# The first expert tile of a fused attention and mixture-of-experts kernel: nine token blocks read back, three picked by one-hot products

## The reference

```python
def reference(**kwargs):
    # 2 batches x 8 heads x 768 tokens x 64: attention only between tokens of one hash bucket
    attn_out = _attn_ref(q, k, v, proj)
    x = attn_out.transpose(0, 2, 1, 3).reshape(1536, 512)
    x = _moe_ref(x, w_in, w_out, a, b)        # g(x @ w_in) @ w_out, d_ff 2048, g a quotient of polynomials
    return _moe2_ref(x, w_gate, w1, w2)       # below

def _moe2_ref(x, w_gate, w1, w2):             # 8 experts, d_ff 1024, one expert per token
    logits = x @ w_gate
    expert_idx = np.argmax(logits, axis=1)
    probs = softmax(logits)
    for e in range(E):
        mask = expert_idx == e
        h = np.maximum(x[mask] @ w1[e], 0.0)
        out[mask] = probs[mask, e][:, None] * (h @ w2[e])
```

## Time and profile before

| | us |
|---|---|
| median of 3 executions | 814.49 (814.44 to 814.61) |
| the profiled execution | 812.37 |
| its span, first to last instruction | 810.5 |
| PE busy | 776.7 (96%) |
| DVE, ACT, POOL busy | 562.9, 492.6, 456.2 |
| mean granted clock of TensorE | 0.987 |

### The profile page before, as it was taken

One profiled execution on the slowest core, in us unless ns is written; L12 is line 12 of the kernel. 1 busy time (PEld: TensorE's weight loads), 2 busy tenths in 40 slices (PEclk: granted clock), 3 DMA queues, 4 the chain that ended last, 5 costly groups with the idle time before them and its releaser, 6 DMA issues.

```text
span 810.5 us, 13370 instructions
## 1 busy us (share of the span) xinstructions
PE 776.7 (96%) x4279; PEld 688.0 (85%) x4279; DVE 562.9 (69%) x966; ACT 492.6 (61%) x975; POOL 456.2 (56%) x404
## 2 busy tenths in 40 slices
PE   6899999999998999999999999995999999999997
PEld 4799899899996889999999999894788888888886
DVE  4788888888896787887778887975354444544451
ACT  4678878878898898778778877954123224222100
POOL 3335265265157687557647654516895659954810
PEclk9999999999999999999999999995999999999999
DMA  8997987975840850960692040074752727561100
GB/s 193 191 218 168 209 168 168 210 167 130 200 154 21 288 186 0 314 220 1 211 356 86 1 186 23 0 223 169 242 192 74 247 68 248 179 234 28 64 36 19
DMA packets 71842, 123.42 MB, mean 152 GB/s; under 512 B 33342, under 2 KB 36126, under 8 KB 67680
## 3 DMA queue, kind: packets, MB, share of 16 engines
q1 hardware_dynamic: 64176, 90.71, 41.9%
q10 hardware_dynamic: 5056, 25.56, 9.4%
q0 software_dynamic: 2544, 6.31, 2.1%
HBM read 60.26 MB, written 34.24 MB: 117 GB/s over the span
## 4 chain that ended last, share of the span: by engine, by line
PE 88%; ACT 5%; issue 3%; DVE 3%; POOL 1%; DMA 1%; POOLq 0%; SPq 0%; ACTq 0%; DVEq 0%
PE ps L1405 7%; PE ps L1493 5%; PE ps L1495 5%; PE ps L1494 5%; PE ps L1527 5%; PE ps L1528 5%; PE ps L1526 5%; PE ps L1671 4%; PE ps L1673 4%; PE ps L1672 4%; PE ps L1697 4%; PE ps L1696 4%; PE ps L1695 4%; PE ps L1417 4%; PE ps L1393 4%; PE ps L1394 4%
## 5 line engine op out<-in xcount | busy, mean ns | idle before, releaser
L789 POOL TENSOR_TENSOR split<-wraw,split 128x512 f32 (+1 forms) x112 | 140.3, 1293 | 53.4 <-ACT split L950 49.9
L950 ACT ACTIVATE split<-wraw 128x512 f32 (+1 forms) x128 | 68.8, 619 | 140.5 <-PE ps L1697 52.0
L1119 DVE TENSOR_TENSOR ptl<-ps,pth 128x512 fp32r<-128x512 f32 x144 | 98.8, 686 | 35.9 <-ACT pth L884 34.1
L764 POOL TENSOR_TENSOR hw<-hw,ha 128x384 f32<-128x384 f32 x64 | 65.4, 1022 | 72.4 <-ACT hw L962 72.4
L884 ACT ACTIVATE pth<-ps 128x512 fp32r<-128x512 f32 x144 | 86.6, 602 | 30.9 <-PE ps L1405 30.7
L1099 DVE TENSOR_REDUCE negmax<-ps 128x1 f32<-128x768 f32 x96 | 91.1, 949 | 6.5 <-PE ps L1394 6.5
L875 ACT ACTIVATE pr<-ps,negmax 128x768 f32<-128x768 f32 x96 | 86.8, 904 | 5.7 <-DVE negmax L1099 5.7
L1405 PE MATMUL ps<-cst,pr 128*128 128x128 f32 x576 | 88.2, 274 | 1.8 <-ACT pr L875 1.8
L1493 PE MATMUL ps<-xh,wih 128*128 128x384 f32 x256 | 86.2, 337 | 1.0 <-DVE hp L1155 1.0
L1495 PE MATMUL ps<-xh,wil 128*128 128x384 f32 x256 | 86.3, 337 | 0.0
L1494 PE MATMUL ps<-xl,wih 128*128 128x384 f32 x256 | 85.9, 336 | 0.0
(11 more groups left out here) (213 smaller groups left out, 2012.7 us busy)
## 6 DMA issues: line engine op xcount, KB each, us to landing
routed<-blank SPq DMA_DIRECT2D x33, 771.0 KB, 14.4
wraw<-in_moe_w ACTq DMA_DIRECT2D x24, 1024.0 KB, 5.5
wraw<-in_moe_w SPq DMA_DIRECT2D x8, 1024.0 KB, 5.7
operand<-qk_hi SPq DMA_DIRECT2D x31, 192.0 KB, 4.5
operand<-qk_hi SPq DMA_DIRECT2D x15, 384.0 KB, 4.9
operand<-qk_lo SPq DMA_DIRECT2D x30, 192.0 KB, 4.3
operand<-mask SPq DMA_DIRECT2D x14, 384.0 KB, 5.3
xg<-routed SPq DMA_DIRECT2D x19, 256.0 KB
```

Source lines behind the costliest of these rows:

```text
L789: pool.tensor_tensor(split_piece(E_LO[x], ring, k), wraw[:, x, i, :], split_piece(E_HI[x], ring, k).bitcast(F32), ALU.subtract).then_inc(e ...
L1119: dve.tensor_tensor(ptl[:, at:at + CW], ps[:, 4 + c % 2, :], pth[:, at:at + CW].bitcast(F32), ALU.subtract).then_inc(ptl_done, 1)
```

## The change

Three things are done.

1. **The first tile's rows.** SP waits for the first nine scatters only (`FIRST_PICK` is 9) and reads the first 128 rows back into `xg`. What blocks 9 to 11 add to these rows is made without DRAM: DVE compares a row of numbers 0 to 127 (`iota`, a new load of 64 KB) with each token's row number, which gives a 128x128 one-hot matrix per block (`pick`), and PE multiplies it with the block's 512 columns in plain float32, three products summed in bank 5 (`gather`). DVE adds the sum to `xg` (`x0_added`). POOL may scatter blocks 9 to 11 only when the early read has landed (`s_x0`), and the gate weights of tile 0 are read later, with tile 1.
2. **High halves first.** In `mm1` the eight products of a half that use only the high part of x come first, and the four with the low part last, so that the first products wait for the high copy alone. For tiles 0 and 1 the high copies are made by ACT (`x_hi`, `h_hi`).
3. **Order.** The queues of PE, DVE and ACT from the last `down` steps on are written in another order, so that chunks 0 to 2 are placed earlier; the work on 48 partitions is put between the halves of `mm1(0)`; five products of 128x512 whose result nobody reads are added (`keep_warm`); the reciprocal of the gate (`gate`) is split off from `choose`; POOL no longer waits for the tables before it splits the second expert's weights.

```diff
+            sp.wait_ge(g_done, NSTEP * M4)
+            sp.dma_start(iota[:, :], consts[:, C_IOTA:C_IOTA + P]).then_inc(s_iota, 16)
             for x in range(2):
                 for c in range(2):
                     load_weights(sp, x, 1, c, STREAM)
...
-                if t == 0:
-                    rows = routed[0:P, :]
...
+                first = sp.value_load(tab_rows[0:1, t:t + 1], min_val=0, max_val=BLANK_TILE)
+                rows = routed_tiles[bass.ds(first, 1), :, :].rearrange("o p r -> (o p) r")
                 sp.dma_start(xg[t % 2][:, :], rows[:, 0:DM]).then_inc(s_xg[t % 2], 16)
+                if t == 1:
+                    sp.wait_ge(xt_ready, 1)
+                    sp.dma_start(gi[:, 0, :], routed[0:P, DM:ROW]).then_inc(s_xg[0], 16)
                 sp.dma_start(gi[:, t, :], rows[:, DM:ROW]).then_inc(s_xg[t % 2], 16)
 
+            sp.wait_ge(s_route, 16 * FIRST_PICK)
+            sp.dma_start(xg[0][:, :], routed[0:P, 0:DM]).then_inc(s_x0, 16)
+            sp.wait_ge(rows_done, 1)
             sp.wait_ge(s_route, 16 * NJ)
-            rows_in(0)
-            sp.wait_ge(rows_done, 1)
             for t in range(1, NSLOT_TILES):
                 rows_in(t)
...
                 for j in range(CT * c, CT * (c + 1)):
+                    if j == FIRST_PICK:
+                        pool.wait_ge(s_x0, 16)
                     pool.indirect_dma_start(out=routed, out_offset=bass.IndirectOffsetOnAxis(ap=slot[:, j:j + 1].bitcast(U32), axis=0),
...
-            pool.wait_ge(table_done, 1)
             for r in range(1, E):
+                if r == 2:
+                    pool.wait_ge(table_done, 1)
...
             act.wait_ge(y_ready, 3 * NSTEP)
-            for x in range(2):
-                weights_hi(x, 1, RING_STEP, range(8))
+            weights_hi(0, 1, RING_STEP, range(8))
+            weights_hi(1, 1, RING_STEP, range(3))
+            x_hi(0)
+            weights_hi(1, 1, RING_STEP, range(3, 8))
+            act.wait_ge(mm1_done, 2)
+            x_hi(1)
+            act.wait_ge(s_route, 16 * NJ)
+            h_hi(0, 0)
+            h_hi(0, 1)
...
+            dve.wait_ge(s_iota, 16)
+            dve.wait_ge(slot_done, 7)
+            for i in range(CT):
+                dve.tensor_scalar(pick[:, i, :], iota[:, :], slotf[:, FIRST_PICK + i:FIRST_PICK + i + 1], None, ALU.is_equal).then_inc(pick_done, 1)
...
+            gate(3)
+            dve.wait_ge(picked_x, 1)
+            dve.wait_ge(s_x0, 16)
+            dve.tensor_tensor(xg[0][:, :], ps[:, PICK_BANK, :], xg[0][:, :], ALU.add).then_inc(x0_added, 1)
...
+                if t >= 2:
+                    dve.tensor_copy(xth[:, :, :], turned).then_inc(xt_hi, 1)
+                dve.wait_ge(xt_hi, t + 1)
+                dve.tensor_tensor(xtl[:, :, :], turned, xth[:, :, :].bitcast(F32), ALU.subtract).then_inc(xt_done, 1)
...
                 dve.wait_ge(mm2_done, t + 1)
+                if t == 0:
+                    dve.wait_ge(s_xg[0], 16)
...
+            def gather(j):
+
+                pe.wait_ge(pick_done, j - FIRST_PICK + 1)
+                mm = pe.matmul(ps[:, PICK_BANK, :], pick[:, j - FIRST_PICK, :], y[:, j, 0:DM], start=(j == FIRST_PICK), stop=(j == NJ - 1))
+                if j == NJ - 1:
+                    mm.then_inc(picked_x, 1)
+
+            def keep_warm(n):
+
+                some = split_piece(S_W1H, 0, 0)
+                for i in range(n):
+                    pe.matmul(ps[:, 4, :], some[:, 0:P], some, start=True, stop=True)
...
+            logit(0)
             down(NSTEP - 2, 2, first)
-            logit(0)
             turn_y(2)
-            down(NSTEP - 2, 2, second)
             logit(1)
             turn_y(3)
+            logit(2)
+            down(NSTEP - 2, 2, second)
...
+            pe.wait_ge(e_lo[0], 8)
+            keep_warm(3)
             ranks(3)
             pe.wait_ge(scum_done, NJ)
-            pe.wait_ge(slot_done, 4)
-            pe.matmul(ps[:, 3, 12 * E:13 * E], cst[:, C_ONE:C_ONE + P], scum[:, NJ, :], start=True, stop=True).then_inc(total_ready, 1)
+            pe.wait_ge(slot_done, 6)
+            pe.matmul(ps[:, 7, 12 * E:13 * E], cst[:, C_ONE:C_ONE + P], scum[:, NJ, :], start=True, stop=True).then_inc(total_ready, 1)
+            keep_warm(2)
+            gather(9)
+            gather(10)
...
 
-                pe.wait_ge(s_xg[t % 2], 32 * (t // 2 + 1))
+                if t:
+                    pe.wait_ge(s_xg[t % 2], rows_landed(t))
+                else:
+                    pe.wait_ge(x0_added, 1)
...
-                pe.wait_ge(xt_done, t + 1)
+                pe.wait_ge(xt_hi, t + 1)
                 for c in range(2):
                     wait(pe, hs_done, 2 * t - 1 + c)
                     for kt in range(KD):
                         k = KD * c + kt
                         pe.matmul(ps[:, c, :], xth[:, kt, :], weights(S_W1H, t, k), start=(kt == 0), stop=False)
-                        pe.matmul(ps[:, c, :], xtl[:, kt, :], weights(S_W1H, t, k), start=False, stop=False)
-                        mm = pe.matmul(ps[:, c, :], xth[:, kt, :], weights(S_W1L, t, k), start=False, stop=(kt == KD - 1))
+                        pe.matmul(ps[:, c, :], xth[:, kt, :], weights(S_W1L, t, k), start=False, stop=False)
+                    if t == 0:
+                        (segments_2, segments_4)[c]()
+                    if c == 0:
+                        pe.wait_ge(xt_done, t + 1)
+                    for kt in range(KD):
+                        mm = pe.matmul(ps[:, c, :], xtl[:, kt, :], weights(S_W1H, t, KD * c + kt), start=False, stop=(kt == KD - 1))
                     mm.then_inc(mm1_done, 1)
+                    if t == 0 and c == 0:
+                        segments_3()
```

More of the change, by code:

```diff
@@ L1205, in choose, with gate @@
                     dve.wait_ge(scum_done, j + 1)
+            def gate(c):
+                js = slice(CT * c, CT * (c + 1))
                 dve.wait_ge(ex_done, c + 1)
@@ L1582, in _ @@
             turn_y(1)
+            logit(0)
             down(NSTEP - 2, 2, first)
-            logit(0)
             turn_y(2)
-            down(NSTEP - 2, 2, second)
             logit(1)
             turn_y(3)
+            logit(2)
+            down(NSTEP - 2, 2, second)
+            turn_y(4)
+            logit(3)
             down(NSTEP - 1, 0, first)
-            logit(2)
-            turn_y(4)
-            down(NSTEP - 1, 0, second)
-            logit(3)
+            ranks(0)
             turn_y(5)
-            down(NSTEP - 1, 1, first)
-            ranks(0)
             logit(4)
             turn_y(6)
+            logit(5)
+            down(NSTEP - 1, 0, second)
+            turn_y(7)
+            logit(6)
+            down(NSTEP - 1, 1, first)
+            ranks(1)
+            turn_y(8)
+            logit(7)
             down(NSTEP - 1, 1, second)
-            logit(5)
-            turn_y(7)
+            logit(8)
             down(NSTEP - 1, 2, first)
-            logit(6)
-            turn_y(8)
+            turn_y(9)
+            ranks(2)
+            turn_y(10)
             down(NSTEP - 1, 2, second)
-            ranks(1)
-            logit(7)
-            turn_y(9)
-            logit(8)
-            turn_y(10)
             logit(9)
@@ L1643, in _, with segments_2, segments_3 @@
-            pe.matmul(ps[0:1, 7, 320:320 + E], order[on, 1:2], chosen[on, :], start=True, stop=True).then_inc(seg_pe, 1)
+            gather(11)
+            def segments_2():
+                pe.wait_ge(seg_dve, 2)
+                pe.matmul(ps[on, 2, 128:128 + NSEG], spread(span[on, 0:1]), cst[on, C_ID:C_ID + NSEG], start=True, stop=True)
+                pe.matmul(ps[on, 2, 192:192 + NSEG], spread(span[on, 1:2]), cst[on, C_ID:C_ID + NSEG], start=True, stop=True).then_inc(seg_pe, 1)
+            def segments_3():
+                pe.wait_ge(seg_dve, 3)
+                pe.matmul(ps[0:1, 7, 192:192 + NTAB], cst[on, C_ONE:C_ONE + 1], placed[on, :], start=True, stop=True)
+                pe.matmul(ps[0:1, 7, 224:224 + NTAB], seg[on, G_RING:G_RING + 1], inside[on, :], start=True, stop=True).then_inc(seg_pe, 1)
@@ new lines, in segments_4 @@
+            def segments_4():
+                pe.wait_ge(seg_dve, 4)
+                pe.matmul(ps[0:1, 7, 256:256 + NTAB], order[on, 0:1], inside[on, :], start=True, stop=True)
+                pe.matmul(ps[0:1, 7, 288:288 + E], seg[on, G_EXPERT:G_EXPERT + 1], chosen[on, :], start=True, stop=True)
+                pe.matmul(ps[0:1, 7, 288 + E:288 + 2 * E], seg[on, G_RING:G_RING + 1], chosen[on, :], start=True, stop=True)
+                pe.matmul(ps[0:1, 7, 320:320 + E], order[on, 1:2], chosen[on, :], start=True, stop=True).then_inc(seg_pe, 1)
```

106 lines of the change are left out of this document (55 added, 51 removed).

## The result

The changed kernel takes **831.37 us** (median, 829.83 to 835.18) against 814.47 us before, measured beside it: ratio 1.0221, 95% interval 1.0200 to 1.0243. The forecast was 808.3 us and its range ended at 813.3. The sign was wrong.

The account below looks back on a forecast made before the run. The prediction took the expert stage as a closed queue of PE work that ends earlier as it begins earlier. Parts 2 to 4 gave -6.0 to -6.4, taken as -6.2: 814.49 - 6.2 = 808.3 us, range 806.8 to 813.3.

Parts of the forecast that it names:

- What bounds the kernel: Expert stage: one closed queue of PE work, so the span moves with the second tile's first product, before at 576.91.
- Part 1: Routing on PE, reordered: idle 2.2 us before logit 0, last logit unchanged at 552.6, chunk 2 placed at 548.5, not 551.6.
- Then the queue is closed again: PE behind the 2.2 us idle before logit 0: no further waits, last logit ends at 552.6, no gain and no loss.
- clock rival: Either rival with a falling clock: near 553 (chance 0.28), or already at 549.9 (chance 0.09).
- Part 2: Picked rows: comparisons 0.2 us each, three gathers 0.94 each; sum for x from 559.1 to 559.8, early read covered.
- Rival A: Clock falls near 553, returns at 560: +2.5, 810.8; falling again before tile 0's products: 812.5 to 813.3; chance 0.28.
- Part 3: Tile 0, high halves first: the first product waits for the high copy alone, 561.2 against 567.16, 6.0 us earlier.
- Part 4: Second tile: tables inside mm1(0), PE idle 1.9 us for a small read, first product 570.5 against 576.91, 6.4 earlier.
- the streams behind: Expert weights behind tile 1: POOL starts its pieces at 561.4 against 562.83, needs 19.9 us; covered with 14 us left.
- tile 4, the first that can use it: Third expert's first matrix: complete at 594, its first user tile 4 comes at 608, so 14 us are left.
- Rival C: Expert stage: the expert weights bound it once PE comes earlier, so the gain doesn't reach the end; 813.1, chance 0.10.
- Rivals A and B: The second: clock falls at 549.9, stays down until 570.4, costing 8.5 against a gain of 6.2; 816.8, chance 0.09.

Follow-up runs that it names:

- c: The changed kernel plus eight products nobody reads, filling PE's hole before logit 0; 827.79 us, ratio 1.0173.
- f: As e, without the eight filling products, logit 0 again behind the half column as in the kernel before; 811.89 us, ratio 0.9982.
- l: As j, with the one DVE operation that stood there also led through PSUM; 810.64 us, ratio 0.9970.
- m: As l, with the products of g among the last logits; 810.97 us, ratio 0.9962.
- e: As d, but DVE makes the eight low pieces of the second expert's first matrix instead of POOL; 810.60 us, ratio 0.9971.
- b: The kernel before, with POOL splitting the second expert's weights without waiting for the tables; 831.61 us, ratio 1.0218.
- a: The changed kernel, with POOL again waiting for the tables before splitting the second expert's weights; 823.29 us, ratio 1.0116.
- d: The changed kernel with the edits of both a and c; 819.65 us, ratio 1.0080.
- g: As f, with six products of 512 columns around the last two logits; 812.14 us, ratio 0.9989.
- h: The kernel before, with POOL making four low pieces of the second expert ahead of its wait for the tables; 816.22 us, ratio 1.0033.
- j: As c, with DVE's table operations rewritten so that none reads two tensors in SBUF; 823.28 us, ratio 1.0126.
- k: As b, with the same rewriting of DVE's table operations as j; 828.20 us, ratio 1.0187.

## Why the prediction was wrong, point by point

- **What bounds the kernel: right.** A closed queue from the second tile on (227.91 against 228.07 us busy), and the span moved with its first product (+22.96 against +22.9).
- **Part 1, the idle before logit 0: right in size, wrong in consequence.** Forecast 2.2, measured 2.21. The step that failed is "Then the queue is closed again": the hole and the order behind it, logits and transposes close together, went with a fall of the clock at 528, more than 20 us earlier than either clock rival placed it (549.9 and 553). The last logit ended at 559.95 instead of 552.6. Filling the hole gave back 3.6 us of the median (c against the changed kernel). The idle time is not the whole cause, since the clock also fell in f with 0.82 us of it, and filling is no sure remedy: in the profile of l the clock was down from 538 to 542.
- **Part 2, the gathers: right on price, short on the clock.** 0.94 us each was taken; at full clock in m two take 1.99 and one 1.13, up to its end. In the changed kernel two take 3.78 (1.89 each, at 1.2 GHz). The comparisons took 0.23 each against 0.2, and the early read was in before the last gather, as forecast, though late: POOL's next scatter waited for it until 565.98, 10.6 us behind chunk 2's row numbers (555.37), where the forecast had 8.9. The Trainium skill, "FP8 and Floating Point Precision", section TensorE Precision Notes, gives true float32 four passes; the rows come within a tenth of it at both levels, a little above: 1.99 for two against eight products of 0.23, and 3.78 for two against eight of 0.43 (1.84 and 3.44).
- **From the last logit to tile 0's first product**: forecast 8.6. Measured 12.8 in the changed kernel and 553.31 to 564.20 = 10.9 in e, where ranks and gathers still ran mostly at 1.2 GHz. This is Rival A's first half ("ranks, products and gathers cost +2.5"), and it did happen: 2.3 in e, where the clock was at half level from 553 until it came back at 559.7, and 4.2 in the changed kernel, where it stayed down from 562 to 575.
- **Part 3, high halves first: right.** The first product follows the transposes with 0.78 us of idle for ACT's copy, and no DVE operation stands between.
- **Part 4, from tile 0 to tile 1**: forecast 9.3; measured 574.21 - 564.20 = 10.0 in e, with the forecast new wait on the small read in it (1.07, forecast 1.9). So the step itself was sized well.
- **Part 4, "the streams behind": the step that failed.** POOL's start was judged only by when its pieces are finished ("POOL comes forward by 1.4 us only"), at no cost. What it runs beside was not asked. Before, its first piece began at 562.83, right behind DVE's last table operation, and never beside one. That left the trace of before nearly silent on the price (the one sign is in the last section), and the prediction left the sum at zero where it should have set bounds: the whole burst, 19.9 us, was the upper one. What the runs showed in its place is a stall of 17.03 us in DVE, of which PE stood for 13.00. That it suffices is shown by b (one edit to the kernel before, +17.4) and by l against c (the same stall avoided in another way, -16.5).
- **The same step again, "tile 4, the first that can use it"**: that is the third expert. The second expert's pieces, needed by tile 1, had a margin of 4.1 us. By the prediction's own figures POOL came forward by 1.4 and PE by 6.4, so 0.9 us of waiting was already in them: the eighth piece at 561.4 + 19.9/2 = 571.4, the product at 570.5. Hidden behind the larger stall in the changed kernel, it shows as soon as POOL waits (6.9 us in a, 7.0 in d). It is Rival C at another place than the one looked at.
- **Rivals A and B** had the clock right as a danger, but placed its first fall too late and priced it too low: the changed kernel fell twice before the first tile's products, and again behind the stall. The prediction held the row at 549 to agree with a fall after idleness. It does not: PE is busy all of that microsecond, as it is at 528 in the changed kernel.

What is left between e and the forecast (a gain of 2.7 us by the medians, against 6.2) can be placed in e's profiled execution, where tile 1 starts 3.7 us later than forecast (574.21 against 570.5): 0.7 at the last logit, 2.3 from there to tile 0's first product (1.3 of them in the first two gathers, 3.26 against 1.99 in m), 0.7 inside tile 0. What makes the clock fall at 528, and in one execution for longer than in the next, stays open, and so does the exact border of the DVE form: the 48x1 operation passed and the 48x8 one stood, and size and kind of operation were not varied apart.

## What to carry to other kernels

When a change lets an engine start earlier, look not only at when its results are wanted but at what the other engines do during its whole burst, above all VectorE and GpSimd. Here small table work on VectorE was kept clear of GpSimd by leading one side of each operation that stood through PSUM. For each buffer that a moved consumer reads, work out the margin of the first consumer, not of the one that is easiest to find; and a few cheap products among narrow TensorE work can be worth more than they cost (3.6 us in c), but need not be: in g and m no gain was shown in eight to ten executions.

## What was not expected of the hardware

A VectorE operation of 0.2 us stood for 17.03 (the changed kernel), 20.20 (b), 5.58 (h), 13.41 (j) and 18.02 us (k) beside GpSimd's operations of 128x512 on SBUF, each time to the end of the whole queue of them (sixteen of them, in h four). Small operations with an input or the result in PSUM, a reduction of 48x48, and operations on one number per partition with one tensor input ran beside the same burst at their usual 0.15 to 0.27 us. GpSimd's own pieces kept their pace: 19.61 us for sixteen, against 19.88 before. The Trainium skill, "SBUF — State Buffer", section "SBUF: two separate sides", says that VectorE and GpSimd share one pair of ports to SBUF as an exclusive lock, which a VectorE operation wants if it has two SBUF inputs or runs in a mode that uses both ports; whichever starts first has the pair for its whole instruction, and the other fully blocks. The forms that stood and passed here agree with the first half, as far as this section tells them apart. The length does not agree with one instruction: here it is the whole burst.

In b the operation started 0.62 us before the first piece (559.31 against 559.93), while POOL was still in its last scatter, and did not end either, though it usually takes 0.21. The trace of before has a small sign of the same:

```profile
558.37 0.96 POOL L795 DMA_INDIRECT routed<-y,slot  x1 [0.30 <-issue]
...
558.95 0.36 DVE L1273 TENSOR_SCALAR inside<-cst,span 48x20 f32<-48x20 f32 x1
```

This operation ends within 0.02 us of the scatter; with POOL idle, in a, it takes 0.22. The one in front of it ran 0.21 beside the same scatter, so which part of a scatter holds DVE up stays open.

How long the clock is at half level differs between executions of one kernel: f ranges from 808.95 to 818.19 us, with a mean granted clock of 0.995 in the quickest and 0.980 in the slowest.
